# A feed-forward of seven block products: a new order of the products, no GpSimd in it, and u prepared during mixing

## What is computed

```python
# 1 decayed linear attention, per batch and head
state = alpha_t[:, None] * state + outer(k_t, v_t);  x_t = q_t @ state        # -> x: 4 x 768 x 384
# 2 mixing
theta = x @ w_theta;  zr, zi = x * cos(theta), x * sin(theta)
u = x + w_tok_r @ zr + w_tok_i @ zi                                           # over the 768 tokens
u = u + relu(u @ w_ch)                                                        # w_ch: 384 x 384
# 3 feed-forward
h = relu(u @ w_in)                                                            # w_in: 384 x 1024
conv = conv_w[0] * h[t-1] + conv_w[1] * h[t] + conv_w[2] * h[t+1]
out = (h * sigmoid(conv)) @ w_out                                             # w_out: 1024 x 384
```

## Time and profile before

| | us |
|---|---|
| median of 3 runs | 555.63 |
| lowest, highest | 552.54, 556.3 |
| the profiled execution's own time | 553.43 |
| its span, first to last instruction | 551.7 |
| its mean granted TensorE clock | 0.988 of full |

### The profile page before, as it was taken

The page is one execution under the profiler, slowest core; times in us unless marked ns, Lnnn a source line. Parts: engine busy times, 40 slices in busy tenths (PEclk is TensorE's granted clock), DMA queues, the critical chain, the costliest instruction groups (busy, mean ns, idle before and its releaser), DMA issues.

```text
span 551.7 us, 10504 instructions
## 1 busy us (share of the span) xinstructions
PE 520.1 (94%) x4022; PEld 501.3 (91%) x4022; DVE 436.5 (79%) x640; ACT 310.7 (56%) x551; POOL 217.4 (39%) x150
## 2 busy tenths in 40 slices
PE   8999999999999999999999798899969996999996
PEld 7989997999999989999999797789869986999996
DVE  8999998998977588667869477688759776887883
ACT  4889888555444443543343644556645565557663
POOL 5999981000001330300017507472647346643320
PEclk9999999999999999999999899899989998999999
DMA  8999979996613122133400021120112011001102
GB/s 329 320 331 339 334 259 239 301 287 124 235 44 66 21 86 87 29 58 126 163 0 1 0 87 43 44 86 1 43 44 86 2 43 45 0 1 43 44 1 86
DMA packets 36994, 61.74 MB, mean 112 GB/s; under 512 B 6096, under 2 KB 25552, under 8 KB 36432
## 3 DMA queue, kind: packets, MB, share of 16 engines
q1 hardware_dynamic: 33824, 56.35, 31.9%
q10 hardware_dynamic: 3120, 4.72, 2.3%
HBM read 46.90 MB, written 14.16 MB: 111 GB/s over the span
## 4 chain that ended last, share of the span: by engine, by line
PE 59%; POOL 15%; issue 13%; DVE 6%; ACT 3%; DMA 1%; SPq 1%; ACTq 0%; POOLq 0%; DVEq 0%
PE y_bank L1809 25%; PE y_bank L1840 6%; PE x_bank L1796 6%; PE y_bank L1891 5%; POOL z L1056 4%; PE weighed L1716 4%; PE x_sum L1674 4%; POOL rest_w L1015 3%; POOL u_part L1056 2%; PE theta_bank L1877 2%; PE x_sum L1689 2%; PE x_bank L1877 2%; PE turned L1701 1%; POOL first_w L1015 1%; DMA q_in<-in_q_rows 1%
## 5 line engine op out<-in xcount | busy, mean ns | idle before, releaser
L1809 PE MATMUL y_bank<-rest_w,z 128*128 128x384 f32 x432 | 78.0, 339 | 2.7 <-DVE z L1476 2.7
L1809 PEld LDWEIGHTS y_bank<-rest_w,z 128*128 128x128 f32 x432 | 76.5, 191 | 3.0 <-DVE z L1476 3.0
L1809 PE MATMUL y_bank<-first_w,z 128*128 128x384 f32 x432 | 76.9, 334 | 0.3 <-issue 0.3
L1809 PEld LDWEIGHTS y_bank<-first_w,z 128*128 128x128 f32 x432 | 75.0, 188 | 0.4 <-issue 0.4
L1000 POOL TENSOR_TENSOR in_w<-out_rows,in_w 128x1024 fp32r<-128x1024 f32 (+1 forms) x4 | 7.4, 1840 | 123.1 <-ACT in_w L1195 123.1
L1171 ACT ACTIVATE sine<-angle 128x384 f32<-128x384 f32 x24 | 12.6, 526 | 55.0 <-DVE angle L1451 55.0
L1840 PE MATMUL y_bank<-u_part,channel_w 128*128 128x384 f32 x216 | 40.7, 337 | 1.8 <-DVE u_part L1518 1.8
L1796 PE MATMUL x_bank<-theta_w,x_t 128*128 128x384 f32 x216 | 41.6, 335 | 0.3 <-DVE x_t L1433 0.3
L1840 PEld LDWEIGHTS y_bank<-u_part,channel_w 128*128 128x128 f32 x216 | 37.5, 188 | 2.9 <-DVE u_part L1518 2.9
L1796 PEld LDWEIGHTS x_bank<-theta_w,x_t 128*128 128x128 f32 x216 | 37.7, 188 | 0.8 <-DVE x_t L1433 0.8
L1891 PE MATMUL y_bank<-first_w,z 128*128 128x384 f32 x144 | 30.6, 340 | 5.8 <-POOL z L1056 4.9
(11 more groups left out here) (208 smaller groups left out, 1339.8 us busy)
## 6 DMA issues: line engine op xcount, KB each, us to landing
a_in<-in_a_rows SPq DMA_DIRECT2D x15, 390.0 KB, 5.9
k_in<-in_k_rows SPq DMA_DIRECT2D x15, 384.0 KB, 5.9
q_in<-in_q_rows SPq DMA_DIRECT2D x14, 384.0 KB, 5.2
v_in<-in_v_tokens SPq DMA_DIRECT2D x16, 288.0 KB, 4.4
x_blocks<-x_scratch SPq DMA_DIRECT2D x12, 288.0 KB, 5.9
u_scratch<-u_sum ACTq DMA_DIRECT2D x6, 576.0 KB, 3.5
out_rows<-u_scratch SPq DMA_DIRECT2D x3, 1152.0 KB, 5.1
y<-x_even SPq DMA_DIRECT2D x6, 576.0 KB, 3.0
```

Of the source, the lines that this page charges most:

```text
L1809: ins = pe.matmul(y_bank[2 * d + half][:, 0:HALF], z[s % 2][part][zp][:, d * P:(d + 1) * P], mixing_w(part, wp, s)[:, half_tokens(half)], ...
```

## The change

`STAGES` now names for each stage its bank, whether it opens a new sum there, and its products. The order is such that p1, u2 = p1 + s2 t2, u3 = u2 + s3 t3 and the first odd half = u3 + a22 t4 + ... pile up in bank 0; ACT copies p1, u2, u3 out on the way. DVE has four additions instead of six. The order of the lists of ACT and DVE in a step, and of the back groups (odd tile first), changes with it.

`split_g` is DVE's in all steps; POOL only clears four columns at the start. The low parts of w_out are made on DVE in the last iteration of mixing instead of on POOL. The block differences of w_in move from batch 1's last iteration to batch 2's first two, and the weight parts behind them one iteration later.

u is no longer stored raw. In batch b + 1 of mixing, ACT rounds and DVE splits and combines batch b's u, straight from `u_sum` into `u_part` (which the channel product no longer needs); SP stores the parts, 2.0 MB in iteration 2 and 1.6 MB in iteration 4, and loads them into place later: batch 0's in the last batch of mixing, batch 1's at the start of the feed-forward, batch 2's in step 2. The last batch's parts are made in steps 0 to 8 and stay on the chip.

```diff
-STAGES = ((("a11", "b11"),), (("s2", "t2"),), (("a12", "b21"), ("even", "c0")), (("s3", "t3"),), (("s1", "t1"),),
-          (("a22", "t4"), ("odd", "c0")), (("s4", "b22"), ("even", "c1")), (("odd", "c1"),))
-BETWEEN = (2, 1, 1, 2, 2, 2, 1, 1)
-BETWEEN_LAST = (1, 1, 1, 1, 1, 1, 1, 1)
-BETWEEN_FIRST = ((0, 0, 2, 2, 1, 1, 1, 2), (2, 1, 1, 1, 1, 1, 1, 1))
+STAGES = ((0, True, (("a11", "b11"),)), (1, True, (("a12", "b21"), ("even", "c0"))), (0, False, (("s2", "t2"),)),
+          (1, True, (("s1", "t1"),)), (0, False, (("s3", "t3"),)), (0, False, (("a22", "t4"), ("odd", "c0"))),
+          (1, False, (("s4", "b22"), ("even", "c1"))), (0, True, (("odd", "c1"),)))
+BETWEEN = (1, 1, 1, 1, 3, 1, 1, 3)
+BETWEEN_LAST = (1, 1, 1, 1, 2, 1, 1, 0)
+BETWEEN_FIRST = ((0, 0, 1, 2, 2, 1, 1, 2), (1, 1, 1, 1, 2, 1, 1, 1))
...
 # mix_batch
+            if b:
+                do.prepare_u(b - 1, s, 0)
...
+            if b:
+                do.prepare_u(b - 1, s, 1)
...
 # SyncE
+        def prepare_u(b, s, spot):
+            if (s, spot) == (2, 1):
+                u_split.done(sp, b, 3)
+                for hl in range(2):
+                    sp.dma_start(b_scratch[b, :, hl, :], u_part[hl][:, 0, half_tokens(0)].bitcast(F32)).then_inc(plain_saved.sem, 16)
+                    sp.dma_start(u_scratch[b, 0, hl, :, :, :], u_part[hl][:, 1:3, :].bitcast(F32)).then_inc(plain_saved.sem, 16)
+            if (s, spot) == (4, 1):
+                u_split.done(sp, b)
+                for hl in range(2):
+                    sp.dma_start(u_scratch[b, 1, hl, :, :, :], u_part[hl][:, 0:2, :].bitcast(F32)).then_inc(sums_saved.sem, 16)
...
 # ScalarE
         def round_u(b, m):
             if m == 0:
-                u_got.done(act, b)
-                h_made.done(act, FF_PAIRS * (b - 1) - 1)
-            if m == 2:
+                multiplied.done(act, b)
+                out_done.done(act, b)
+            if m == 3:
                 u_combined.done(act, b)
+                if b < LAST:
+                    plain_saved.done(act, b)
...
+        def prepare_u(b, s, spot):
+            for m in {(0, 1): (0, 1), (1, 1): (2,), (3, 1): (3,), (4, 0): (4,)}.get((s, spot), ()):
+                round_u(b, m)
...
         def sums_of(b):
             multiplied.before(act, b, 1)
+            sums_saved.done(act, b - 1)
             for half in range(2):
                 round_sums(b, half)
...
         def begin(n):
             if n == 0:
                 multiplied.before(act, LAST, 1)
+                sums_saved.done(act, LAST - 1)
                 round_sums(LAST, 0)
...
         def step(k):
...
+            if makes:
+                keep_p1(n)
+            if shapes:
+                relu_even(m, 1)
+                conv1(m, 0)
+            if makes:
+                relu_even(n, 0)
+                keep_u2(n)
+            if shapes:
+                gate(m, 1)
...
+            if makes:
+                keep_u3(n)
...
+            if shapes:
+                gate(m, 0)
+                round_g(m, 1)
+            if makes:
+                relu_odd_first(n)
+            if shapes:
+                round_g(m, 0)
...
+            if makes:
+                relu_odd_second(n)
+                conv1(n, 1)
...
 # VectorE
+        def prepare_u(b, s, spot):
+            for m in {(1, 0): (0,), (1, 1): (1,), (2, 0): (2,), (4, 0): (3,), (4, 1): (4,)}.get((s, spot), ()):
+                split_part(b, m)
+            for i in {(2, 1): (0,), (3, 0): (1,), (3, 1): (2, 3)}.get((s, spot), ()):
+                combine(b, i)
...
         def step(k):
...
+            if 0 <= k < FF_STEPS - 1:
+                split_g(k, 0)
+            if shapes:
+                conv2(m, 1)
+            if makes:
+                gather_even_first(n)
+            if shapes:
+                conv3(m, 1)
...
+                conv2(m, 0)
+                conv3(m, 0)
+            if makes:
+                gather_c22(n)
+            if shapes:
+                apply_gate(m, 1)
+                apply_gate(m, 0)
+                split_g(m, 1)
...
+            if makes:
+                gather_odd_second(n)
+                gather_even_second(n)
...
 # TensorE, stage(n, i): what it waits for before writing
-            if i == 2:
-                p1_kept.done(pe, n)
-            if i == 4:
-                even_first.done(pe, n)
+            if i == 2:
+                kept.done(pe, n, 1)
+            if i == 4:
+                kept.done(pe, n, 2)
             if i == 5:
+                kept.done(pe, n, 3)
+            if i == 7:
+                kept.done(pe, n, 4)
```

More of the change, by code:

```diff
@@ L233 @@
 scan_state high bring keep low theta_high theta_low compare waves refill refill_v judge place divert decide store store_half store_late halve flip lower theta angle sines
-product round_z fill load load_blocks load_first blocks_first load_weight spare prepare mix sums end send begin step""".split()
+product round_z fill load load_blocks load_first blocks_first load_weight spare prepare prepare_u mix sums end begin step""".split()
 Work = namedtuple("Work", PLACES, defaults=[nothing] * len(PLACES))
@@ L372, in mix_batch @@
             tile(do.round_z, b, s + 1, last)
-            if s == T - 1 and not last:
-                do.send(b, 0)
             if b == 0:
@@ L627, in layer @@
     multiplied, out_done = tally("multiplied", 6, 1), tally("out_done", 6, 1)
-    u_stored = [tally(f"u_stored{half}", 16, 1) for half in range(2)]
-    assert BATCH - 1 == MODEL_TILES
     w_got, w_high, w_low, w_added, out_w_got, out_w_high, out_w_low, taps_got, last_stored = (
@@ L948, in _ @@
         program(sp, Work(refill_piece=refill_piece, refill=refill, refill_v=refill_v, decide=decide, store=store, store_half=store_half, store_late=store_late,
[L949 removed]
+                         load_blocks=load_blocks, load=load, load_first=load_first, blocks_first=blocks_first, load_weight=load_weight, spare=spare, prepare=prepare, prepare_u=prepare_u, begin=begin, step=step))
         for t in stored:
@@ L1087, in _ @@
         pool.memset(quarter[:, :], PI / 2).then_inc(const, 1)
-        program(pool, Work(scale_q=scale_q, scale_k=scale_k, select=select, spare=spare, prepare=prepare, begin=begin, step=step))
+        program(pool, Work(scale_q=scale_q, scale_k=scale_k, select=select, spare=spare, begin=begin))
     @block.scalar
@@ L1505, in add_u @@
                 x_high.done(dve, b * T + T - 1)
+                u_split.done(dve, b - 1)
             mixed.done(dve, b * T + T - 1, half + 1)
-            u_stored[half].before(dve, b, 1)
             for d in range(MODEL_TILES):
@@ L1535, in end, with split_part, combine @@
                 end_block(b, half, d)
-        def gather_u2(n):
-            p1_kept.done(dve, n)
+        def split_part(b, m):
+            u_rounded.done(dve, b, m + 1)
+            high, low = u_split_of(b, m)
+            dve.tensor_tensor(low, u_sum_of(m), high.bitcast(F32), ALU.subtract).then_inc(u_split.sem, 1)
+        def combine(b, i):
+            first, second, third, fourth = (u_sum[:, d, half_tokens(half)] for d in range(2) for half in range(2))
+            out, left, right = ((first, second, first), (second, fourth, second), (fourth, fourth, first), (third, third, fourth))[i]
+            if i == 0:
+                u_split.done(dve, b, 2)
+            u_combined.done(dve, b, i)
+            dve.tensor_tensor(out, left, right, ALU.subtract).then_inc(u_combined.sem, 1)
@@ L1867, in stage @@
             if i == 4:
-                even_first.done(pe, n)
+                kept.done(pe, n, 2)
             if i == 5:
+                kept.done(pe, n, 3)
+            if i == 6:
                 gathered.done(pe, n, 2)
-            if i == 6:
-                gathered.done(pe, n, 3)
             if i == 7:
-                gathered.done(pe, n, 4)
-            terms = [(ff_w[w][wp][:, q, :], ff_u[u][b % 2][up]) for w, u in STAGES[i] for wp, up in PASSES]
+                kept.done(pe, n, 4)
+            bank, opens, products = STAGES[i]
+            terms = [(ff_w[w][wp][:, q, :], ff_u[b][u][up]) for w, u in products for wp, up in PASSES]
             for m, (w, u) in enumerate(terms):
-                ins = pe.matmul(h_bank[i % 2][:, 0:HALF], w, u, start=m == 0 and i not in (2, 6), stop=m == len(terms) - 1,
+                ins = pe.matmul(h_bank[bank][:, 0:HALF], w, u, start=m == 0 and opens, stop=m == len(terms) - 1,
                                 skip_group_check=True)
```

360 lines of the change are left out of this document (147 added, 213 removed).

## The result

The changed kernel takes 523.73 us (median of 4 runs, 523.15 to 525.06) against 554.24 us (4 runs, 552.54 to 556.30) for the kernel before in the same comparison: ratio 0.9451, 95% interval 0.9407 to 0.9495. The forecast was 529 us, its range 519 to 541. The profiled execution took 525.06 us with a span of 523.3 us. One run of an experiment further down (the store cut in two) took 830.34 us at a mean granted clock of 0.558 and is left out of that kernel's median.

A forecast was written before the change was run, and what follows sets the result against it. PE's matmul pace bounds the kernel, with 29.5 us lost in 13 feed-forward steps. Start 313.6, begin steps 24.1, full steps 157.3 and end 30.0 give 525.0; plus 1.73, 526.7; with factor 1.004, 529 us, range 519 to 541.

The forecast's parts named there:

- start of the feed-forward: When mixing ends: 314.08 less 2.69, 1.70 and 1.19, plus 2 x 2.3 and 0.5, giving 313.6 us.
- begin steps: Two opening feed-forward steps: 20.8 + 2.3 for a store + 1.0 for DVE's work, 24.1 us in all.
- 13 full steps: Feed-forward steps at 12.1 us each, bounds 11.97 and 12.9: 157.3 us against 185.1.
- the end: From the last full step to the end of the span, only the order changes: 30.0 us.
- the 7.4 us off each long step: Feed-forward: no ACT rounding waits for POOL, so 7.4 to 7.5 us over pace go in each long step.
- hand-layout: One step's stages laid out from PE's pace: about 0.8 to 0.9 us to spare at each bank 0 release.
- rivals A and D: Feed-forward steps: A, DVE bounds them at 12.9 us, 539 (0.15); D, PE meets busy ACT at bank 0, 573 (0.03).
- Rival E: Feed-forward: micro-waits pull the clock down, 1.7 us of half clock per step, 22 more, 551 us; chance 0.03.
- So the 2.69 us go, with them 1.7 us, and the 1.19.: Mixing: without batch 0's u work on POOL, the waits at 306.1 and 198.4 and 1.7 us of half clock go.
- 0.5 us, bounds 0 and 5: Mixing, batch 2: weight differences and four weight splits on POOL beside a fuller DVE cost 0.5 us.
- The stores, 2.3 us each, three times: ACT waits for the parts' store to land: 2.3 us in batches 1, 2 and at feed-forward start; bounds 0 and 4.5.
- rival B: Stores land later, waits of 4.5 us with 1.7 of half clock behind each: 11.7 more, 541 us; chance 0.13.

The follow-up runs named there:

- the store cut in two: Changed kernel with w_out's load held until batch 2's sums are rounded, plus the sums' store split into two blocks, each issued once split: 520.92 us, ratio 0.9432.
- two-by-two table: Old or new product order, g splits on POOL or DVE; old order without u work: 527.74 (POOL), 524.26 us (DVE); new: 525.14 (POOL), 523.73 (DVE).
- GpSimd apart: Changed kernel with w_out's load later, POOL's weight differences waiting for batch 1's u and two weight splits one iteration later: 522.70 us, ratio 0.9439.
- the other profile of the changed kernel: The changed kernel run again unchanged, beside three experiment kernels on one chip: 524.98 us, ratio 0.9469.

## Why the prediction was right, and where not

| term | forecast | measured |
|---|---|---|
| start of the feed-forward | 313.6 | 317.06 |
| begin steps | 24.1 | 21.93 |
| 13 full steps | 157.3 | 155.58 |
| the end | 30.0 | 28.73 |
| span | 525.0 | 523.3 |

The main step stands: POOL out of the feed-forward takes the 7.4 us off each long step, and the full steps cost PE's pace. The three stages of the feed-forward were each forecast 1.3 to 2.2 us too long, the start 3.5 too early; on the span these errors cancel to 1.7. The main mechanism was right, and so were most of the smaller ones; that the sum of their sizes came out this close is partly luck. The rest of the 5.3 us lies in the runs: I put a factor of 1.004 on the profiled time, since the median shown of before lay above it, and the median of after lies 1.3 us below its own profiled 525.06.

*The steps.* I took 12.1 for 11.96: I left 0.13 us for late hand-overs and there are none, after the first. The hand-layout was right that each release has room, and rivals A and D are dead: in the steps at pace DVE works up to 10.6 us of 11.97 (11.4 in the first, of 12.07) and PE doesn't wait. Rival E falls as well: five of eight stages go through one bank, and the clock reads 1.00 in every step. The begin steps, of which I said that DVE would hold them by 1.0 us, took 10.96 each.

*What the new order is for.* I counted on it for the hand-overs. The two-by-two table shows that the full steps reach PE's pace without it, if DVE splits g; it brought 2.4 us, nearly all in the begin steps and the first full one.

*"So the 2.69 us go, with them 1.7 us, and the 1.19."* The first two went. The 1.19 did not: it became 1.91. The step assumed that the weight differences, written into batch 2 of POOL's list, would run in batch 2. POOL's list is not paced by the batches; the only thing it waited for was its own third split, so it ran them at 194.1, straight into batch 1's end. "GpSimd apart" shows 1.3 us less there with them gone (2.07 to 0.81), and the cut store takes the rest.

*"0.5 us, bounds 0 and 5" for the weight work beside a fuller DVE.* This is the mis-sized term. It cost 1.26 us at z and 1.3 at batch 1's end, 2.6 us, and up to 4.4 where it was put worse (2.86 and its clock). The other figure I gave, from the rule of the Trainium skill ("SBUF — State Buffer", Who interferes with whom), was 5 us for eight operations, 0.63 each. The 3.2 us by which four operations lengthened DVE are 0.8 each. In the changed kernel four of the eight met DVE, two at each place, and lengthened it by 1.25 and 1.52 us, 0.7 each. I took the low value because no row showed such a meeting. For one operation that meets DVE the rule was near; the 2.6 us in all lie halfway between my two figures, since the other four lengthened DVE by 0.35 us and PE's wait by nothing.

*The stores, 2.3 us each, three times.* At batch 2's end 2.26, as said, but by another sum: the store landed after 6.5 us as forecast, with the w_out load behind it, and alone it takes 5.5. In the third place there was next to nothing (a gap of 0.42 us), since PE has the first stages of the feed-forward to run before it needs ACT. In the first it was hidden partly behind POOL. And I kept the clock at full behind 2.3 us. In this profile it was not: 1.5 us, which rival B had with 1.7. By their mean clocks (0.993, 1.000) it fell more often or not at all in other runs of the same kernel, so no single value would have been right.

The start of the feed-forward by these: the wait at 306.1 gone with its clock, -4.4; batch 1's end +0.7; z +1.3; batch 2's end +2.3 + 1.5. That is +1.4 on 314.08. The measured difference is +3.0; some 0.9 us of the rest lies ahead of mixing, which begins 0.89 us later in this profile (87.55 against 86.66). Stage 1 was not changed, and in the other profile of the changed kernel mixing begins at 86.12, so this is spread between executions. The last 0.7 stays open; I didn't test it.

*The end*, 28.73 for 30.0, where I expected nothing: of the 1.3 us, 0.7 lie behind the last matmul's start (3.38 us instead of 4.05) and 0.4 in the last step's products. Why the part behind the last matmul is shorter was not tested. One wait of PE is left, 0.76 us in front of its first product with a split of DVE (L1585).

## What to carry to other kernels

Work on an engine with time to spare is not free; it costs by what runs beside it: four to eight small operations of GpSimd cost 2.6 to 4.4 us beside VectorE's work on SBUF, and nothing that shows in its pause of 3.3 us. The splits of g show the other side: on GpSimd beside VectorE they cost the full steps nothing in the new order of the products, and 4.7 us (161.0 against 156.3) in the old one. An in-order list with no wait in it runs as early as it can, whatever loop it is written in, so look up when moved work will in fact start. And where an operand buffer is also a store's source, the store's landing stands in the chain: issue it in pieces, each as soon as it is made, with no big load right behind.
